# Opening of an attention stage: the second pair of heads turned once and stacked by ScalarE and DMA, the first head's score rows spread over four PSUM banks

## The reference

```python
scores = scale * np.matmul(q, k.transpose(0, 1, 3, 2))        # 576 x 576 for each of 32 heads
scores = np.where(causal, -1000000000.0, scores)
scores = scores - scores.max(-1, keepdims=True)
a = np.exp(scores); a /= a.sum(-1, keepdims=True) + 1e-09
local = np.matmul(a, v)
q_p = np.where(q > 0, q, np.exp(q) - 1.0) + 1.0                # phi
mem_out = (q_p @ M_prev) / ((q_p @ z_prev)[..., None] + 1e-06)
out = g * mem_out + (1 - g) * local                           # then the two MLPs
```

## Time and profile before

| | us |
|---|---|
| median of 3 runs | 820.97 (820.97 to 821.49) |
| the profiled execution, its own time | 821.17 |
| its span | 819.4 |
| PE busy | 810.7, 99% of the span |
| DVE busy | 510.4, 62% |
| ACT busy | 339.6, 41% |
| POOL busy | 339.1, 41% |

### The profile page before, as it was taken

How to read it: one execution, slowest core, us unless ns; L and a number is a source line. 1 busy time by engine, 2 the same in 40 slices (tenths; PEclk the granted TensorE clock), 3 DMA queues, 4 the chain that set the end, 5 groups by cost and what they waited for, 6 DMA issues and landing times.

```text
span 819.4 us, 14574 instructions
## 1 busy us (share of the span) xinstructions
PE 810.7 (99%) x5630; PEld 704.2 (86%) x5630; DVE 510.4 (62%) x1052; ACT 339.6 (41%) x608; POOL 339.1 (41%) x453
## 2 busy tenths in 40 slices
PE   8999999999999999999999999999999999999998
PEld 7788888888888888888888899999998888888886
DVE  7877777776588653333433353346688977777762
ACT  6766776675422232222322232233436434333431
POOL 6667676676899930000000000005268844443300
PEclk9999999999999999999999999999999999999999
DMA  8587777866134320000000000000111000000001
GB/s 152 128 178 154 173 167 155 178 142 144 53 103 116 95 73 1 1 1 0 1 1 0 1 1 1 1 1 1 52 51 52 26 27 26 26 14 27 26 14 51
DMA packets 86371, 49.45 MB, mean 60 GB/s; under 512 B 65056, under 2 KB 73248, under 8 KB 86304
## 3 DMA queue, kind: packets, MB, share of 16 engines
q1 hardware_dynamic: 83760, 47.94, 24.3%
q10 hardware_dynamic: 2544, 0.59, 0.4%
HBM read 27.28 MB, written 4.72 MB: 39 GB/s over the span
## 4 chain that ended last, share of the span: by engine, by line
PE 96%; DVE 1%; issue 0%; ACT 0%; POOL 0%; POOLq 0%
PE ps_h L1297 8%; PE ps_y L1313 8%; PE ps_h L1298 8%; PE ps_h L1299 8%; PE ps_y L1314 8%; PE ps_y L1312 8%; PE ps_v L678 5%; PE ps_s L591 4%; PE ps_r L1766 4%; PE ps_r L1764 4%; PE ps_r L1765 4%; PE ps_hid L1701 4%; PE ps_hid L1699 4%; PE ps_hid L1700 3%; PE ps_x L657 3%; PE ps_x L658 3%
## 5 line engine op out<-in xcount | busy, mean ns | idle before, releaser
L1414 DVE TENSOR_TENSOR xT<-xT 128x512 f32<-128x512 f32 (+1 forms) x80 | 61.2, 765 | 127.7 <-ACT xT L1372 127.7
L1598 POOL TENSOR_TENSOR win<-stage,win 128x512 fp32r<-128x512 f32 x2 | 2.6, 1296 | 282.4 <-ACT win L1833 282.4
L1314 PE MATMUL ps_y<-g_hi,wout 128*128 128x512 f32 (+1 forms) x320 | 117.5, 367 | 0.0
L1313 PE MATMUL ps_y<-g_lo,wout 128*128 128x512 f32 (+1 forms) x320 | 117.5, 367 | 0.0
L1312 PE MATMUL ps_y<-g_hi,wout 128*128 128x512 f32 (+1 forms) x320 | 117.4, 367 | 0.0
L1378 ACT ACTIVATE g_hi<-xT 128x512 fp32r<-128x512 f32 (+1 forms) x80 | 47.3, 591 | 135.0 <-DVE xT L1416 135.0
L1297 PE MATMUL ps_h<-x_hi,win 128*128 128x512 f32 (+1 forms) x280 | 103.0, 368 | 0.0
L1299 PE MATMUL ps_h<-x_hi,win 128*128 128x512 f32 (+1 forms) x280 | 102.8, 367 | 0.0
L1298 PE MATMUL ps_h<-x_lo,win 128*128 128x512 f32 (+1 forms) x280 | 102.8, 367 | 0.0
L1372 ACT ACTIVATE xT<-ps_h 128x512 f32<-128x512 f32 (+1 forms) x80 | 44.3, 554 | 139.0 <-PE ps_h L1299 137.2
L1419 DVE TENSOR_TENSOR g_lo<-xT,g_hi 128x512 fp32r<-128x512 f32 (+1 forms) x80 | 65.1, 813 | 52.6 <-ACT g_hi L1378 52.6
(11 more groups left out here) (220 smaller groups left out, 1814.6 us busy)
## 6 DMA issues: line engine op xcount, KB each, us to landing
stacked<-cut SPq DMA_DIRECT2D x56, 288.0 KB, 4.8
out<-res SPq DMA_DIRECT2D x18, 256.0 KB, 2.0
v_raw<-in_v SPq DMA_DIRECT2D x32, 128.0 KB, 2.7
stage<-in_moe_w_in SPq DMA_DIRECT2D x16, 256.0 KB, 2.8
stage<-in_moe_w_out SPq DMA_DIRECT2D x16, 256.0 KB, 2.7
k_raw<-in_k SPq DMA_DIRECT2D x28, 128.0 KB, 2.6
q_raw<-in_q SPq DMA_DIRECT2D x28, 128.0 KB, 3.6
stage<-in_moe_w_in SPq DMA_DIRECT2D x4, 512.0 KB, 3.5
```

The lines of the kernel that those rows point to most:

```text
L1313: pe.matmul(out, wout[:, f, HI, w], g_lo[:, r, 0:n], start=False, stop=False)
L1314: ins = pe.matmul(out, wout[:, f, LO, w], g_hi[:, r, 0:n], start=False, stop=(f == FT - 1))
L1414: dve.tensor_tensor(r, r, r, ALU.mult).then_inc(square_done, 1)
```

## The change

What it does, engine by engine:

- Only the first pair is direct (`DIRECT = 1`). The second pair's keys and queries go to `k_raw[1]` and `q_raw[1]`, are turned once (`turn_queries(1)`, then `turn_keys(1)`), and are cut into `cut[1]`: `round_second_queries` and `round_keys(1)` on ACT, `low_second_queries` and `cut_keys(1)` on DVE. `double` on POOL and the second pair's swapped turns on PE are gone.
- Half of the second pair's stack is written by ACT, 64 partitions x 1152 words a head (`third_head`, `fourth_head`); the other half by two DMAs of SP (`stack(1)`). They stand ahead of the values in SP's list, and the values stand ahead of the memory.
- Head 0's tiles 3, 0 and 2 go to the two banks of `ps_x` (`X_AT`), and their waits on `maxed` are gone. Head 0's maxima are transposed after head 1's first rows.
- POOL, not DVE, works out the low part of the queries of head 1 (`low_queries`); the clearing of `K1`'s ones for later pairs (`fill_others`) comes after it. ACT repeats the second pair's queries (`repeat_queries(1, ...)`) between chunks of head 1.
- DVE does `work_out_rest` before head 2's first rows, where it did it after head 3's second.

```diff
-    DIRECT = 2
-    BY_ACT = [(0, "k_own0"), ..., (1, "k_own1"), (1, "q_own1")]
-    BY_DVE = [(0, "k_own1"), (0, "k_moved1"), (0, "q_lo0"), (0, "q_lo1"), (1, "q_lo0")]
+    DIRECT = 1
+    X_AT = {3: (0, 0), 0: (1, 0), 2: (1, P)}
+    BY_ACT = ["k_own0", "k_moved0", "q_hi0", "q_cut0", "q_hi1", "q_own1", "third_head", "fourth_head"]
+    BY_DVE = ["k_own1", "k_moved1", "q_lo0"]
@@ SP: stack(p) and its order
+                if p > 1 or par == 1:
                     sp.dma_start(words(stacked[0:D, to, :, 0:S]), mine[:, Q_HI:K_HI + 1:2, :]).then_inc(arrived, 16)
+                if p > 1 or par == 0:
                     sp.dma_start(words(stacked[D:P, to, :, 0:S]), mine[:, Q_LO:K_HI + 1, :]).then_inc(arrived, 16)
         load_queries(2)
+        stack(1)
+        load_values(0)
         load_memory()
-        load_values(0)
         load_keys(3)
@@ POOL
-        double(first_k[1], k_in[1])
-        double(first_q[1], q_in[1])
-        pool.wait_ge(doubled_pool, 2)
-        repeat_first(0)
+        repeat_first()
         pool.wait_ge(repeated, 1)
         clear_others()
-        repeat_first(1)
-        pool.wait_ge(repeated, DIRECT)
-        spread_maxima(0)
         low_queries()
         pool.wait_ge(low_by_pool, 1)
+        spread_maxima(0)
+        fill_others()
@@ PE
         first_rows(0)
-        turn_swapped_keys(1)
-        pe.wait_ge(qT_copied, 1)
-        keep_warm(ps_t[:, 0:P])
         second_rows(0)
-        turn_keys(1)
-        turn_queries(1)
         third_rows(0)
-        turn_swapped_queries(1)
-
+        turn_queries(1)
+        turn_keys(1)
         first_rows(1)
-        act_placed(pe, 1, "q_hi1")
-        keep_warm(ps_x[MINE[0], 0, 0:P], 4)
+        turn_maxima(0).then_inc(scored, 1)
+        keep_warm(ps_x[:, 0, 0:P])
+
         cross(0, 0)
@@ ACT
+            elif what in ("third_head", "fourth_head"):
+                act.wait_ge(k_hi_done, 1)
+                act.wait_ge((q_hi_done, q_lo_done)[what == "fourth_head"], 1)
+                own, to = ((Q_HI, 2), (Q_LO, 3))[what == "fourth_head"]
+                half = MINE[to - 2]
+                place, source = stacked[half, to, :, 0:S], words(cut[1][half, own:K_HI + 1:K_HI - own, :])
...
+        for what in BY_ACT[:-2]:
+            put(what)
+        copy_queries(0)
+        open_gates()
+        round_second_queries()
+        copy_queries(1)
+        round_keys(1)
+        put("third_head")
         exp_weights(0, 0)
...
         exp_weights(0, 3)
+        put("fourth_head")
         round_keys(2)
...
         feature_exp(1)
+        repeat_queries(1, 0)
+        repeat_queries(1, 1)
         exp_weights(1, 2)
@@ DVE
+        def low_second_queries():
+            dve.wait_ge(q_hi_done, 1)
+            dve.wait_ge(qT_copied, 2)
+            dve.tensor_tensor(cut[1][:, Q_LO, :], qT[1][:, :], cut[1][:, Q_HI, :], ALU.subtract).then_inc(q_lo_done, 1)
...
         first_rows(0)
-        low_queries(0, 1)
         second_rows(0)
-        work_out_gates()
         third_rows(0)
+        low_second_queries()
 
         first_rows(1)
+        work_out_gates()
         second_rows(1)
         third_rows(1)
-        low_keys(1, 0)
+        work_out_rest()
         first_rows(2)
-        low_keys(1, 1)
+        cut_keys(1)
```

More of the change, by code:

```diff
@@ L258, in cut_is_free, with score_rows @@
             stacks_taken(eng, p - 2)
[L259 to L263, removed]
+            if p == 3:
+                act_placed(eng, "fourth_head")
+        elif p == 2:
+            dve_placed(eng, "q_lo0")
+    def score_rows(h, t):
+        if h == 0 and t in X_AT:
+            bank, at = X_AT[t]
+            return ps_x[:, bank, at:at + keys[t]]
+        return ps_s[:, S_AT[t]:S_AT[t] + keys[t]]
     def tiles(eng, raw, a, p, arrived):
@@ L276, in load_keys @@
             need(sp, kT_turned, p - 1)
[L277 removed]
+            tiles(sp, first_k if p < DIRECT else k_raw[p % 2], k, p, k_in[p % 2])
         def load_queries(p):
@@ L588, in rows_of_scores, with turn_maxima @@
             n = keys[t]
+            rows = score_rows(h, t)
             for lo, hi in ((0, min(n, 512)), (512, n)):
                 if lo < hi:
-                    ins = pe.matmul(ps_s[:, S_AT[t] + lo:S_AT[t] + hi],
+                    ins = pe.matmul(rows[:, lo:hi],
                                     stacked[:, a, 0, P * t:P * (t + 1)], stacked[:, a, 1, lo:hi], start=True, stop=True)
             return ins
+        def turn_maxima(h):
+            need(pe, maxed, 4 * (h + 1))
+            return pe.transpose(ps_s[:, NEG_AT:NEG_AT + P], least[h % 2][:, :], ident[:, :])
         def first_rows(h):
@@ L597, in first_rows @@
                 pe.wait_ge(cleared, FOR_ROWS)
[L598 to L611, removed]
+                act_placed(pe, "q_hi1")
+                dve_placed(pe, "q_lo0")
+            elif h == 1:
+                act_placed(pe, "q_own1")
+                pe.wait_ge(low_by_pool, 1)
+                pe.wait_ge(maxed, 2)
             elif h < HEADS:
                 p = h // 2
[L614 to L617, removed]
+                pe.wait_ge(stack_landed[p % SLOTS][h % 2], stack_landed_at(p))
+                if p == 1:
+                    act_placed(pe, ("third_head", "fourth_head")[h % 2])
+            if is_head(h - 1) and h != 1:
+                ins = turn_maxima(h - 1)
             if h < HEADS:
@@ L868, in copy_output, with put @@
             act.activation(xT[:, kt, b * S:(b + 1) * S], ps_t[:, 0:S], ACT.Copy).then_inc(xT_done, 1)
-        def put(p, what):
-            half, to = int(what[-1]), slot(2 * p + int(what[-1]))
+        def put(what):
+            if what[-1] in "01":
+                half, to = int(what[-1]), slot(int(what[-1]))
             if what[:-1] == "k_own":
-                act.wait_ge(kT_turned, p + 1)
-                place, source = stacked[MINE[half], to, 1, 0:S], keys_psum(p)[MINE[half], 0:S]
+                act.wait_ge(kT_turned, 1)
+                place, source = stacked[MINE[half], to, 1, 0:S], keys_psum(0)[MINE[half], 0:S]
             elif what[:-1] == "k_moved":
-                act.wait_ge(swapped_turned, K_SWAPPED[p])
+                act.wait_ge(swapped_turned, K_SWAPPED)
                 place, source = stacked[MINE[1 - half], to, 1, 0:S], \
@@ L975, in vector @@
     def vector(dve):
-        for s in range(2):
-            dve.memset(first_k[s][REST:P, FULL, 0:2, :], 0.0).then_inc(cleared_dve, 1)
-            dve.memset(first_q[s][REST:P, FULL, 0:2, :], 0.0).then_inc(cleared_dve, 1)
+        dve.memset(first_k[REST:P, FULL, 0:2, :], 0.0).then_inc(cleared_dve, 1)
+        dve.memset(first_q[REST:P, FULL, 0:2, :], 0.0).then_inc(cleared_dve, 1)
         dve.memset(ps_v[:, 1, :], 0.0).then_inc(cleared_dve, 1)
@@ L1155, in vector @@
         second_rows(3)
-        work_out_rest()
         third_rows(3)
```

176 lines of the change are left out of this document (79 added, 97 removed).

## The result

| | before | changed |
|---|---|---|
| median of 9 runs (us) | 821.02 (820.72 to 821.49) | 823.37 (822.6 to 824.16) |
| ratio, 95% interval | | 1.0025 (1.0016 to 1.0033) |
| the profiled execution | 821.17 | 822.62 |
| forecast | | 821.4 (819.3 to 822.8) |

The forecast was "no change that can be measured"; the kernel became 2.35 us slower, outside the range; the interval of the ratio, 1.0016 to 1.0033, is clear of 1. The profiled execution of the changed kernel is at the fast end of its nine, only 1.45 above its counterpart.

The account below looks back on a forecast made before the run. PE was taken as the bound, with only the first 48 us movable. Its lead shrank from 2.1 us through 1.4, 0.8 and 0.5 to -0.4 at head 6: 821.17 + 0.4 - 0.2 = 821.4 us, range 819.3 to 822.8.

Parts of the forecast that it names:

- What bounds the kernel: Whole kernel: PE busy 810.7 of 819.4 us; only the first 48 us can move, PE's position there carries through.
- Head 0's scores: Opening: DVE's five maxima of head 0 follow each other and end at 13.75, 1.6 us earlier.
- the new waits on POOL, ACT and DVE: Opening: POOL's costs nothing, with 0.15 to spare; the one on ACT and DVE costs 0.35 us before negT.
- g: PE's position against the kernel before, positive meaning ahead; forecast 2.1 us at cross(0, 0), -0.4 at head 6.
- DVE's keys: Before head 0's values: both halves of pair 2's key cut come behind head 2's rows, costing 0.75 of g.
- SP: SP's list: stack(1) waits until 14.55, then 12.3 us of issues; stack(2) 1.2 later at 28.2, memory lands at 25.4.
- `stack(2)` and `stack(3)`, slack at heads 4 and 6: Late stack DMAs hold PE: g = 0.5 at head 4; 0.8 us of slack exceeded at head 6, g = -0.4.
- The clock: Rival: PE's new waits before head 0's values and memory halve the clock for 4 us, costing 2 us: 823.4; chance 0.03.
- SP falls further behind: Rival: issues behind the stack's transfers lengthen, stack(2) starts at 29.2 to 30, 1.4 to 2.2 us lost: 822.8; chance 0.13.

Follow-up runs that it names:

- e6: e1 with DVE's key cut of the second pair in two halves and the gates' work later: 819.38 us, 0.9977 of the kernel before.
- e1: Changed kernel with the memory's four DMAs ahead of the second pair's stack in SP's list: 820.47 us, 0.9986 of the kernel before.
- e4: Changed kernel with head 0's score rows back in two banks, with the waits on the maxima: 824.57 us, 1.0043 of the kernel before.
- e10: Changed kernel with DVE's key cut in two halves and the gates' work later, SP's order left: 824.02 us, 1.0030 of the kernel before.
- e11: Changed kernel unaltered, run again for a second profile: 822.95 us, 1.0026 of the kernel before.
- e7: Kernel before, with SP waiting for head 0's copied maxima before values and memory, values first: 821.60 us, 1.0002 of the kernel before.
- e9: Kernel before, memory and values 0 in their old place, rest of SP's list held until head 0's last exponential: 821.52 us, ratio 1.0001.
- e8: Kernel before, SP's list held until head 0's maxima are spread, values ahead of memory: 822.15 us, 1.0009 of the kernel before.
- e2: Changed kernel with SP's order stack(1), memory, values 0: 825.87 us, 1.0054 of the kernel before.
- e12: Changed kernel with eight identity matmuls on PE just before head 0's memory product: 822.00 us, 1.0005 of the kernel before.
- e5: e1 with head 0's score rows back in two banks: 821.55 us, 1.0002 of the kernel before.

## Why the prediction was wrong, step by step

- **What bounds the kernel** (PE, only the first 50 us count, what PE is behind there is behind at the end): right, by the last column of the table.
- **Head 0's scores, the new waits on POOL, ACT and DVE:** right. The last maximum ended at 13.36 (forecast 13.75; PE had begun 0.2 earlier), `negT` began at 14.31 (14.5), cross(0, 0) at 15.79 (15.8). The earlier start is in these numbers: counted from head 0's rows g was 1.96, not 2.16, so the exact hit on 15.8 is in part luck. A 1152-column copy took 1.16 (1.15). One cost was missing, see the last section.
- **DVE's keys:** right in kind, a wait of 0.60 for 0.75. e6, which takes most of it away, is 0.9 faster than e1 (each against its own before), with the gates' work moved as well.
- **SP, the step that failed first.** The mechanism (a waiting DMA in mid-list delays the memory) was right, its size not. The forecast had the memory landing at 25.4, in a wait of about 0.6; it landed at 26.85, in one of 2.12. The memory's issues began at 18.66 (forecast 18), and landing came 8.2 after that instead of 6.8. Of these 1.4 us the memory's four issues are 1.2 (one took 2.26), and the last transfer, 4.51 for 4.3, is 0.2; the forecast had allowed 0.6 for both. I had taken the spans of the old list. That the stack's 0.6 MB of transfers lengthen what is issued behind them is likely but not shown alone: the values' three issues took 2.9 us, up to the next issue, behind the stack (changed, e1, e4, e6, e10, e11) and 2.1 to 2.3 without it (before, e7, e9), but 2.8 in e8, which has no stack there either, and the memory's 2.26 was 0.77 in e4. g was -0.7 instead of +0.8: 1.5 us of the miss.
- **`stack(2)` and `stack(3)`, slack at heads 4 and 6:** wrong. `stack(2)` was at 29.14, close to its late bound (29.2), and `stack(3)` at 42.78, but neither PE nor anyone waits at head 6 (48.45 is 0.7 late, all from the memory). The step that failed is the landing time: 5.3 carried over from the earlier trace rows, where the second DMA of `stack(3)` took 4.4 in the changed kernel (43.44 to 47.8) and 4.7 in e7, in time for head 6 in both. The consumer that I left out is not a reader of the stack: ACT's rounding of pair 5's keys reuses `cut`, and with it come DVE's key cut and PE's output turn. It waits for the *last* of four DMAs, where I had looked at the first two. The end at 822.62 holds 0.9 of this.
- **The clock, the rival given 0.03.** I argued against it with 0.44 us idle in 4 us, and did not ask what a memory later than forecast would do to that. With 2 us idle ahead of the memory product the clock was lower in 6 of 9 executions (7 of 11 in e11). Its price, 2 us for 4 us at half clock, was too high: the runs show some 0.8 for e11's 4 us at 0.62 and 0.53, and 2.1 for e2's 6 us at 0.50. I called it 823.4, and that the median was 823.37 is luck: the rival had the clock fall on top of a forecast of 821.4, and in the run the two waits alone give 1.45 over 821.17, with 0.75 more to the median in executions at a lower clock. The failed step was to treat the two rivals as separate. "SP falls further behind" brings about "the clock".

**What stays open.** `stack(3)`'s last DMA lands 7.0 us after its issue in the changed kernel's first profile and 4.4 to 5.0 in e9 and e12, with the same bytes. Most of that is when the last issue gets through (6.4 in the kernel before): from the first of the four issues to the last landing it is 9.2 us in the changed kernel, 8.65 before, 8.1 in e9 and e12. What makes the remaining difference no run tells, so the share of the 0.9 wait in a typical execution isn't known. Why the same 2 us of idle PE lowers the clock in some executions and not in others isn't shown either. The wait alone isn't the condition: e8's profile has one of 2.08, and all eleven of its executions had a mean clock of 0.999 or 1.000. There PE had been busy 5.6 of the 6 us from 20 to 26, in the changed kernel 3.7 of them. Nor was a version tried that starts the memory earlier still or gives the stack its own queue.

## What to carry to other kernels

A DMA that waits for a semaphore in the middle of an in-order list delays all that stands behind it, here by 1.1 us more than the wait (a list of 13.4 us for 12.3); put what is ready and needed soon ahead of it. For each transfer that moves, list also who may *overwrite* its source, and count from its last DMA. When a wait of PE grows from 0.4 to 2 us, as here, its own length may not be the whole cost: look at the granted clock in the stretch behind it, in more than one execution, and if the wait can't be removed, try filling it with matmuls, which kept the clock at 1.000 in eleven of eleven executions here.

## What the runs showed of the hardware that was not expected

**DVE beside a memset of POOL.** In the changed kernel DVE's 128 x 40 `tensor_scalar` (SBUF to SBUF) takes 1.45 us:

```profile
15.53 1.53 POOL L375 MEMSET K<- 64x1728 f32 x1
15.65 1.45 DVE L1001 TENSOR_SCALAR inv_gate<-exp_beta 128x40 f32<-128x40 f32 x1
```

The same instruction took 0.18 in the kernel before, at 13.8, and 0.22 in e6, at 20.7. Here it ends at 17.10, the memset that began 0.12 ahead of it at 17.06. It kept DVE from head 1's next maximum for some 0.6 us (PE had written that tile's rows by 16.83, DVE began at 17.46), which the forecast didn't have. In e6 and e10 DVE's key cut stands in its place, a `tensor_tensor` with one input in PSUM: it began 0.12 after the same memset too and took its usual 0.74 and 0.75. So the instruction beside the memset decides. The Trainium skill, "SBUF — State Buffer", section "Who interferes with whom", says that VectorE and GpSimd share a pair of SBUF ports, that `tensor_scalar` is among the instructions that can take it, and that whoever is issued first holds it for the whole instruction while the other blocks fully; the trace agrees, with 0.04 us between the two ends, also in e1 and e5.

**Issue and landing under load.** An issue on SP took 0.6 usually; behind the stack's two transfers one of the memory took 2.26, and the two of the values' first row 2.15 together. A 4 KB transfer of the memory landed 3.8 to 6.4 us after its issue across the runs, and 288 KB after 3.3 to 7.3. The Trainium skill, "DMA: Bandwidth & Descriptors", section "Anatomy of one DMA — SWDGE (gpsimd) path", fits about 2.0 us fixed plus the bytes at 436 GB/s to single DMAs that GpSimd issues, an estimated 2.0 and 2.7 us for these two. The DMAs here are issued by SP and have others in flight, so no run here tests that fit; it is no price for them.
